# A fused retention, top-1 expert and top-2 attention kernel: the gathers behind the experts wait for tile halves, places are turned sooner, constants are multiplied in TensorE's waits

## The reference, cut to what matters

```python
# 1: retention, 8 heads of 64
for t in range(S):
    state = gamma * state + outer(k[:, :, t], v[:, :, t])
    y[:, :, t] = scale * q[:, :, t] @ state
# 2: one expert of 8 per token; a token keeps the expert of the one before it unless it is "fresh"
for b in range(B):
    for s in range(S):
        fresh_e = argmax(logits[b, s])
        e = fresh_e if s == 0 or local_gate[b, s] < 0.5 else prev_e
        prev_e = e
        out[b, s] = softmax(logits[b, s])[e] * (relu(x[b, s] @ w1[e]) @ w2[e])   # 512 -> 1024 -> 512
# 3: causal attention in each of 4 experts (head width 64), the best 2 of them mixed for each token
for e in range(4):
    a = softmax(causal(scale * (x @ wq[e]) @ (x @ wk[e]).T))
    out += weight_of_e_in_top2 * (a @ (x @ wv[e]) @ wo[e])
```

## Time and profile before

| | |
|---|---|
| median of 3 runs | 441.63 us (440.08 to 442.58) |
| the profiled execution | 441.96 us, of which the span of its instructions 440.4 us |
| PE busy | 400.6 us (91%), 3,224 matmul records |
| PEld | 357.2 us (81%) |
| DVE | 250.3 us (57%) |
| ACT | 230.3 us (52%) |
| POOL | 79.0 us (18%) |
| chain that ended last | PE 74%, issue 10%, DMA 7% |

### The profile page before, as it was taken

The page is one execution under the profiler, slowest core; times in us unless marked ns, Lnnn a source line. Parts: engine busy times, 40 slices in busy tenths (PEclk is TensorE's granted clock), DMA queues, the critical chain, the costliest instruction groups (busy, mean ns, idle before and its releaser), DMA issues.

```text
span 440.4 us, 9525 instructions
## 1 busy us (share of the span) xinstructions
PE 400.6 (91%) x3224; PEld 357.2 (81%) x3225; DVE 250.3 (57%) x483; ACT 230.3 (52%) x502; POOL 79.0 (18%) x100
## 2 busy tenths in 40 slices
PE   6999995397999999999999996599899899989987
PEld 5888783296999999999989895499787789978875
DVE  1576778775474746464646454335877441586740
ACT  4866665154464646464646462135666452466643
POOL 1011112011010101010000000730288300025330
PEclk9999998589999999999999999599999999999999
DMA  8958795777877776767767921542200030220003
GB/s 267 347 187 278 248 392 185 243 254 244 287 260 248 262 258 237 279 240 264 250 202 267 328 102 45 150 137 74 71 1 2 2 115 29 71 71 0 0 0 143
DMA packets 32354, 77.55 MB, mean 176 GB/s; under 512 B 3834, under 2 KB 4090, under 8 KB 32330
## 3 DMA queue, kind: packets, MB, share of 16 engines
q1 hardware_dynamic: 25642, 58.28, 39.2%
q0 software_dynamic: 4224, 14.68, 9.7%
q10 hardware_dynamic: 2464, 4.27, 2.7%
HBM read 56.18 MB, written 17.89 MB: 168 GB/s over the span
## 4 chain that ended last, share of the span: by engine, by line
PE 74%; issue 10%; DMA 7%; POOL 2%; DVE 2%; ACT 2%; SPq 1%; POOLq 1%; ACTq 0%; DVEq 0%
PE bank L1239 7%; PE bank L1240 7%; PE bank L1241 7%; PE bank L1226 6%; PE bank L1224 6%; PE bank L1225 6%; PE bank L1343 5%; PE bank L1328 5%; PE bank L1310 3%; PE bank L1314 3%; PE bank L1285 3%; PE bank L1284 3%; PE bank L1286 3%; POOL tokens_by_expert L448 2%; DMA tokens_by_expert<-zero 2%
## 5 line engine op out<-in xcount | busy, mean ns | idle before, releaser
L1224 PE MATMUL bank<-xh,w1h 128*128 128x240 f32 x256 | 71.1, 278 | 0.9 <-DVE xl L904 0.9
L1225 PE MATMUL bank<-xl,w1h 128*128 128x240 f32 x256 | 70.9, 277 | 0.0
L1226 PE MATMUL bank<-xh,w1l 128*128 128x240 f32 x256 | 70.8, 277 | 0.0
L898 DVE TENSOR_TENSOR w2l<-raw,w2h 128x1024 fp32r<-128x1024 f32 x32 | 37.2, 1221 | 42.7 <-ACT w2h L582 42.6
L582 ACT ACTIVATE w2h<-raw 128x1024 fp32r<-128x1024 f32 x32 | 31.7, 1051 | 47.8 <-PE bank L1241 45.7
L1239 PE MATMUL bank<-w2h,hh 128*128 128x512 f32 x128 | 50.6, 395 | 0.0
L1224 PEld LDWEIGHTS bank<-xh,w1h 128*128 128x128 f32 x256 | 49.4, 193 | 1.3 <-DVE xl L904 1.0
L499 POOL TENSOR_SCALAR att<-att,stat,mixw 128x128 f32<-128x128 f32 (+5 forms) x48 | 34.1, 719 | 88.9 <-DVE stat L1054 88.9
L1240 PE MATMUL bank<-w2l,hh 128*128 128x512 f32 x128 | 49.9, 390 | 0.0
L1241 PE MATMUL bank<-w2h,hl 128*128 128x512 f32 x128 | 49.8, 389 | 0.0
L1225 PEld LDWEIGHTS bank<-xl,w1h 128*128 128x128 f32 x256 | 49.4, 193 | 0.3
(11 more groups left out here) (161 smaller groups left out, 863.3 us busy)
## 6 DMA issues: line engine op xcount, KB each, us to landing
raw<-in_w SPq DMA_DIRECT2D x64, 512.0 KB, 6.2
tokens_by_expert<-zero POOLq DMA_DIRECT2D x8, 512.0 KB, 6.5
xr<-tokens_by_expert POOLq DMA_DIRECT2D x8, 512.0 KB, 4.2
kt_in<-in_kT SPq DMA_DIRECT2D x12, 256.0 KB, 4.9
q_in<-in_qT SPq DMA_DIRECT2D x12, 256.0 KB, 3.5
out<-osb SPq DMA_DIRECT2D x12, 256.0 KB, 2.0
outputs_by_expert<-zero SPq DMA_DIRECT2D x6, 480.0 KB
v_in<-in_vR SPq DMA_DIRECT2D x11, 256.0 KB, 4.2
```

What stands on the lines that cost most here:

```text
L898: dve.tensor_tensor(part(low), raw[:, q, :], part(high).bitcast(F32), ALU.subtract).then_inc(w_lo, 1)
L1224: pe.matmul(to, w1h[:, dc, at], xh[:, dc, 0:TILE], start=(dc == 0), stop=False)
L1225: pe.matmul(to, w1h[:, dc, at], xl[:, dc, 0:TILE], start=False, stop=False)
L1226: last = pe.matmul(to, w1l[:, dc, at], xh[:, dc, 0:TILE], start=False, stop=(dc == DC - 1))
```

## The change

- **Places.** Behind the last block TensorE multiplies the places of group 4 before the gates of block 11, and VectorE reads them before it counts group 5.
- **Constants.** TensorE multiplies constants (or weights that lie there) into PSUM bank 0, which nobody reads: two fp32 products of 256 columns behind the last gates, two behind the places of group 5, sixteen (`BUSY`) behind the counts, two (`BETWEEN`) behind the small product of the tile offsets; and ten and four fp32r products of 512 columns (`STILL`) ahead of the first and the second turning at the attention layer's entry.
- **Value products** follow the turning by one block, and not by two.
- **Padding.** GpSimd waits for SyncE's `first_padded` behind its own padding store, ahead of the tile load.
- **Stores.** Each half has its own semaphore `ey_stored[th]`. The zero stores (seven instead of six) have another, `ys_cleared`, for which ScalarE waits once, before the first expert. ScalarE no longer waits for all stores at the end: GpSimd does.
- **Gathers.** The last expert's count at the end of sequence 0 is kept (`seq_count`, `seq_row`), and VectorE works out for each half how many tiles have to be stored before sequence 0 can be gathered (`seq_i`). GpSimd reads these two numbers and waits for them; behind the six gathers it waits for all stores and raises `all_stored`, for which ScalarE and VectorE wait ahead of the attention's loop.

```diff
@@ -37,9 +37,12 @@
...
 WARM = 6
+BUSY = 16
+BETWEEN = 2
+STILL = (10, 4)
 GROUPS = ((0, 2), (2, 4), (4, 6), (6, 8), (8, 10), (10, 11), (11, 12))
 GMAX = 2
-CLEARED = MAX_TILES - E
+CLEARED = MAX_TILES - E + 1
@@ -54,7 +57,9 @@
...
 C_PADMIN = C_PICK + 1 + E
-C_N = C_PADMIN + E
+C_HALVES = C_PADMIN + E
+MAXH = -(-S // TILE)
+C_N = C_HALVES + TH * MAXH
@@ -96,6 +101,8 @@
...
     small[:, C_PADMIN] = TW
+    small[:, C_HALVES:C_HALVES + TH * MAXH] = (TILE * np.arange(MAXH)[None, :] + P * np.arange(TH)[:, None]).reshape(-1)
+    small[:, C_HALVES] = -1.0
     return decay.astype(np.float32), small.astype(np.float32)
@@ -139,6 +146,10 @@
...
         over = sb("over", [1, E * MAXT])
+        seq_count = sb("seq_count", [E, 1])
+        seq_row = sb("seq_row", [1, 1 + TH])
+        seq_over = sb("seq_over", [1, TH * MAXH])
+        seq_i = sb("seq_i", [1, TH], I32)
         ones = sb("ones", [E, GMAX * P])
@@ -241,7 +252,10 @@
...
         ey_done, ey_ready = sem("ey_done"), sem("ey_ready")
-        ey_stored, all_stored = sem("ey_stored"), sem("all_stored")
+        ys_cleared, all_stored = sem("ys_cleared"), sem("all_stored")
+        ey_stored = [sem(f"ey_stored{th}") for th in range(TH)]
+        seq_counted, seq_step, seq_ready, seq_stored = (
+            sem("seq_counted"), sem("seq_step"), sem("seq_ready"), sem("seq_stored"))
         delta_ready, pos2_step, pos2_ready = (
@@ -397,9 +411,9 @@
...
             sp.wait_ge(zeroed, 1)
-            for g in range(E, MAX_TILES):
-
-                sp.dma_start(rows(ys, g * TILE, TILE).rearrange("(p a) n -> p (a n)", p=TILE // 2), zero[0:TILE // 2, :]).then_inc(ey_stored, 16)
+            for g in range(MAX_TILES - CLEARED, MAX_TILES):
+
+                sp.dma_start(rows(ys, g * TILE, TILE).rearrange("(p a) n -> p (a n)", p=TILE // 2), zero[0:TILE // 2, :]).then_inc(ys_cleared, 16)
             for s in range(XRING):
@@ -457,7 +471,6 @@
...
             pool.wait_ge(first_tile_in, 16)
-            pool.wait_ge(first_padded, 16)
             pool.wait_ge(route_ready, 1)
@@ -471,16 +484,23 @@
...
                         pool.wait_ge(padded, 16 * e + 16)
+                        pool.wait_ge(first_padded, 16)
                     pool.wait_ge(tileT_done, 2 * g + 2)
                     load_tile(r)
+                return tb, nt
...
                 expert_loads(e, True)
-            expert_loads(E - 1, False)
+            tb, nt = expert_loads(E - 1, False)
             pool.wait_ge(pos2_ready, 1)
-            pool.wait_ge(all_stored, 1)
+            pool.wait_ge(seq_ready, 1)
+            tiles = [pool.value_load(seq_i[0:1, th:th + 1], min_val=E - th, max_val=MAX_TILES) for th in range(TH)]
+            for th in range(TH):
+                pool.wait_ge(ey_stored[th], 16 * tiles[th] + 16)
+            pool.sem_inc(seq_stored, 1)
+            pool.wait_ge(seq_stored, 1)
             def gather(b):
@@ -490,6 +510,10 @@
...
             gather(0)
+            for th in range(TH):
+                pool.wait_ge(ey_stored[th], 16 * (tb + nt) + 16)
+            pool.sem_inc(all_stored, 1)
+            pool.wait_ge(all_stored, 1)
             gather(1)
@@ -592,21 +616,24 @@
...
-                act.wait_ge(ey_stored, 16 * CLEARED + 16 * TH * (n - 1))
                 for th in range(TH):
                     live = min(P, TILE - th * P)
+                    act.wait_ge(ey_stored[th], 16 * n)
                     act.wait_ge(ey_done, TH * (n - 1) + th + 2)
...
                                              "there are at most MAX_TILES tiles, and n is at least one")
-                    act.dma_start(rows(ys, row, live), ysb[0:live, th, :]).then_inc(ey_stored, 16)
+                    act.dma_start(rows(ys, row, live), ysb[0:live, th, :]).then_inc(ey_stored[th], 16)
...
             act.activation(exps[:, :, :], exps[:, :, :], ACT.Exp).then_inc(exps_ready, 1)
+            act.wait_ge(ys_cleared, 16 * CLEARED)
+            for th in range(TH):
+                act.sem_inc(ey_stored[th], 16)
@@ -637,8 +664,6 @@
...
             tile_out(act.snap(tb + nt))
-            act.wait_ge(ey_stored, 16 * CLEARED + 16 * TH * (tb + nt))
-            act.sem_inc(all_stored, 1)
@@ -650,11 +675,12 @@
...
-            for t in range(C + 2):
+            for t in range(C + 1):
                 if t < C:
                     split_x2(0, t)
-                if t >= 2:
-                    values(0, t - 2)
+                if t >= 1:
+                    values(0, t - 1)
+            act.wait_ge(all_stored, 1)
             with act.Fori(0, B) as b:
@@ -818,6 +844,8 @@
...
                     dve.wait_ge(places_done, g - 1)
+                if g == closing[C - 1]:
+                    dve.tensor_copy(seq_count[:, :], cnt[:, s, w - 1:w]).then_inc(seq_counted, 1)
                 dve.scalar_tensor_tensor(post[:, s, 0:w], cnt[:, s, 0:w], cst[0:E, C_EBASE:C_EBASE + 1], sel[:, s, 0:w],
@@ -848,10 +876,10 @@
...
             last = len(GROUPS) - 1
+            read_places(last - 2)
             count_places(last - 1)
...
             fresh_choice(last)
-            read_places(last - 2)
             read_places(last - 1)
@@ -903,6 +931,7 @@
...
+            dve.tensor_copy(seq_row[:, 0:1], bank[0:1, 6, 2 * E - 1:2 * E]).then_inc(seq_step, 1)
             for q in range(4):
@@ -933,6 +962,15 @@
...
                                      ALU.add).then_inc(pos2_ready, 1)
+
+            dve.wait_ge(seq_step, 1)
+            dve.tensor_tensor(seq_over[:, :], seq_row[:, 0:1].to_broadcast([1, TH * MAXH]),
+                              cst[0:1, C_HALVES:C_HALVES + TH * MAXH], ALU.is_gt).then_inc(seq_step, 1)
+            dve.wait_ge(seq_step, 2)
+            dve.reduce_sum(seq_row[:, 1:1 + TH], seq_over[:, :].rearrange("o (h k) -> o h k", h=TH), AX.X).then_inc(seq_step, 1)
+            dve.wait_ge(seq_step, 3)
+            dve.tensor_tensor(seq_i[:, :], seq_row[:, 1:1 + TH],
+                              route_f[:, R_TB + E - 1:R_TB + E].to_broadcast([1, TH]), ALU.add).then_inc(seq_ready, 1)
@@ -974,6 +1012,7 @@
...
                 split_x2(0, t)
+            dve.wait_ge(all_stored, 1)
             with dve.Fori(0, B) as b:
@@ -1183,15 +1222,24 @@
...
                     block_kv(i)
+            def keep_clock(n):
+
+                for _ in range(n):
+                    pe.matmul(bank[:, 0, 0:2 * P], ident, cst[:, 0:2 * P], start=True, stop=True)
+
             last_g = len(GROUPS) - 1
             turn_fresh(last_g - 1)
+            turn_places(last_g - 2)
             rows_and_gates(NB - 1)
-            turn_places(last_g - 2)
+            keep_clock(2)
             turn_fresh(last_g)
             turn_places(last_g - 1)
+            keep_clock(2)
             turn_places(last_g)
             ends = (GROUPS[last_g][1] - GROUPS[last_g][0]) * P
+            pe.wait_ge(seq_counted, 1)
             pe.wait_ge(cnt_ready, last_g + 1)
+            pe.matmul(bank[0:1, 6, E:2 * E], seq_count[:, :], ident[0:E, 0:E], start=True, stop=True)
             pe.matmul(bank[0:1, 6, 0:E], cnt[:, last_g % 2, ends - 1:ends], ident[0:E, 0:E], start=True, stop=True).then_inc(counts_done, 1)
@@ -1204,11 +1252,13 @@
...
+            keep_clock(BUSY)
             pe.wait_ge(first_tile_in, 16)
...
             pe.matmul(bank[:, 7, 0:E], ones[0:1, 0:P], over[0:1, 0:E], start=True, stop=True).then_inc(ey_done, 1)
+            keep_clock(BETWEEN)
             pe.wait_ge(spare_set, 2)
@@ -1263,13 +1313,15 @@
...
-            for t in range(C + 2):
+            for t in range(C + 1):
+                for _ in range(STILL[t] if t < len(STILL) else 0):
+                    pe.matmul(bank[:, 0, :], hh[:, 0, 0:P], w2h[:, 0, :], start=True, stop=True)
                 if t < C:
                     turn_x2(0, t)
-                if t == 2:
+                if t == 1:
                     pe.wait_ge(m2_lo, 2)
-                if t >= 2:
-                    project_values(0, t - 2)
+                if t >= 1:
+                    project_values(0, t - 1)
             pe.wait_ge(masks_set, 2)
```

## The result

The changed kernel takes 435.23 us (median of 4 runs, 434.74 to 435.92), the kernel before 441.0 beside it (440.08 to 442.58); the ratio is 0.9867, 95% interval 0.9832 to 0.9901 (it is formed from runs beside each other, and need not be the quotient of the two medians). That is 5.8 us faster. The forecast was 429.0, a gain of 12 from there, and its range ended at 434: the direction was right, the size was not.

What follows compares the result with a forecast made beforehand. TensorE was taken as the bound nearly everywhere, with gains only where it waits or runs at half clock: routing to second expert tile (5.2 us) and experts' end (7.7). Together 12.9 off 441.96 gave 429.0 us, range 426.5 to 434.

Steps and rivals of the forecast that it cites:

- Part 1: End of routing: places turned sooner let the last scatter start earlier; 0.4 us taken, bounds 0 and 0.8.
- Part 2: Ahead of the first expert tile: fillers keep TensorE's clock up, so the first layer ends 3.1 us sooner.
- Rival (a): Fillers ahead of the first tile start at half clock and end late: 430.7 us, about 435.7 if slow throughout; chance 0.20.
- the sign of being wrong: Second expert tile waits for its load as long as before, or a new wait follows the gathers.
- Part 3: Second expert tile: GpSimd's earlier padding store lets its load go sooner, taking 5 us; its transposes come 5.2 us earlier.
- Rival (b): Second tile's load shares the DMA engines, takes its old 8.2 us, lands at 100.3: 432.1 us; chance 0.11.
- the first place: Stretch from routing to the second expert tile, where TensorE waits or runs at half clock; forecast gain 5.2 us.
- Part 4: End of experts: gathers wait only for halves holding sequence 0; first gather starts at 270.45 instead of 275.88, 5.4 us.
- The sign given: End of experts: first gather seen at about 265.3 in the changed profile, 270.45 less 5.2.
- Rival (c): End of experts: first gather still waits for the second half, so nothing gained there: 436.4 us; chance 0.03.
- Part 5: Attention layer's entry: fillers and shorter lag keep the clock; projections 7.7 us sooner, 5.4 from the gather, 2.3 the clock.

Runs made afterwards that it cites:

- e1: Changed kernel with GpSimd's wait for SyncE's first padding put back ahead of its own padding store; 438.85 us, ratio 0.9918.
- e3: Changed kernel with SyncE's w1 loads for expert 1 held until the second tile's rows have landed; 434.29 us, ratio 0.9824.
- e10: Changed kernel with the second padding store issued early by SyncE behind the first tile's load, GpSimd's later ones an expert further ahead; 427.66 us, ratio 0.9737.
- a_again: The changed kernel once more, nothing altered; 434.72 us, ratio 0.9898.
- e8: Changed kernel with old order of places, no fillers ahead of the first tile and the padding wait put back; gathers' changes stay; 433.39 us, ratio 0.9854.
- b_again: The kernel before once more, nothing altered, for a second profile; 444.2 us in one run.
- e4: Changed kernel without the constant products around the first tile (two, two, sixteen and two); 439.19 us, ratio 0.9874.
- e6: Changed kernel with the first gather waiting for all halves of all tiles, as in the kernel before; 444.88 us, ratio 1.0034.
- e9: Changed kernel with the value products again two blocks behind the turned blocks instead of one; 437.46 us, ratio 0.9943.
- e2: Changed kernel with each GpSimd padding store one expert further ahead, the first before its wait for the first tile; 433.62 us, ratio 0.9799.
- e7: Changed kernel with GpSimd's paddings one expert further ahead and no constant products around the first tile; 435.41 us, ratio 0.9794.

## Why the prediction was wrong, point by point

- **Part 1** (taken 0.4 us, 0 to 0.8): the step came, and then brought nothing. From xT to the last scatter it is 6.69 us (66.84 to 73.53), before 7.54 (69.38 to 76.92): 0.85, just over the upper bound. But the scatter then took 3.79 us and not 2.99, and the first tile was turned 14.3 us behind xT, as before. In e1 and e3 the scatter took 2.87 and 3.15, and the tile came at 13.5 and 13.6. Why it was slower in the changed profile, no run shows.
- **Part 2**, fillers: right in mechanism. The clock reads 1.00 through them, sixteen and their neighbours end at 80.3 and the tile comes 0.8 us behind; the first layer starts 2.72 us behind the first transposes (81.14 to 83.86; 2.62 forecast). Rival (a) didn't come. TensorE was ready for the second tile 28.0 us behind xT, before 30.4: 2.4 us of the 3.1 forecast (the rest is part 1's 0.4, and a first layer of 11.0 us instead of 10.8). They were won and then lost: TensorE was ready at 94.9 and waited 5.30, twice the 2.56 of before. The prediction had named just that as the sign of being wrong.
- **Part 3 is the step that failed**, in three terms. The padding store had bounds of 4.2 and 6.2 us and took 7.53: the forecast added two for "the weight loads in flight", and the store ran beside four w2 loads that had started only 4.0 us before it (80.09; 6.35 us before it in the old trace). The w1 loads were left at "about 93", their old place, though they follow the same first tile and moved with it, to 90.89. And so the tile load, issued at 92.45 within its bounds, didn't go ahead of them: 5 us taken, 7.68 measured, near the other end (8.2). It landed at 100.13, forecast 97.2. The end of the forecast's own bounds (93.3 + 8.2 = 101.5) held it; the choice within them, "because most of the weight loads start behind it", was wrong in its reason: two of the four were issued ahead of it. What ended the wait instead was that load beside its neighbours: e3 takes the neighbours away and it takes 4.15 us, with 1.78 of wait.
- **What the wait did to the clock** was in no term. A rest of 5.30 us before the second tile cost about 1 us in its transposes (1.97 against 1.10 in the earlier trace rows and 0.87 for the third) and slowed the products until about 104.7 (0.43 us from one to the next, then 0.23). From the second tile's transposes to the third's it is 24.8 us (100.18 to 124.95) where e10 takes 22.5 (94.74 to 117.26): 2.3 us, the last of the gain (1.4 in a_again's profile, 23.9 us). The kernel before isn't safe from it either: behind rests of 2.56 us in its first profile and 2.81 in e8 the second tile's transposes ran at the full clock (1.10 us), behind 2.51 in b_again and 2.91 in e4 at the half one (1.97), which is most of why the third tile of the kernel before stands at 55.5 in one profile and at 57.4 in the other. Rival (b) had the landing right (100.3) but not the store and not the clock: 2.1 us left for the first place, 432.1 in all; in truth nothing was left. The Trainium skill's rule that it drew on (Trainium Kernel Development and Optimization, Key Constraints: transfers from the three queues run on the same 16 DMA engines and interleave) fits what e3 shows here: 7.68 us beside the weight loads, 4.15 without.
- **Part 4**, the gathers: right. The first gather went at 270.31, forecast 270.45. (The sign given, 265.3, took the first place's 5.2 us off, which didn't come; the last expert tile was turned at 259.99 in both profiles.) e6 shows that it rests on the first half. Rival (c) didn't come.
- **Part 5**: mechanism right, size 1.2 us short (7.7 forecast, 6.5 measured). Its first transposes came at 274.25, forecast 274.5. The term that failed is the spacing of blocks, taken as 1.46 us from the old gathers, so that a step of TensorE, 1.88, was the bound: the third and fourth steps took 2.51 and 2.14, 0.9 of the 1.2. The third gather was issued at 272.90, 0.16 us behind the last half's store (272.74), and took 5.24 us against 3.48. In a_again, e8, e9 and e10, issued as close behind that store, it took 4.8 to 5.4. That the store is the reason isn't shown: other gathers are in flight beside it too, and no run takes the store away.
- **What the first place can give.** With the load out of the weights' way e10 has a span 5.7 us shorter than e8, which lacks the first place (431.9 and 426.2), and 5.7 by the medians; forecast 5.2. e10's ratio of 0.9737 is near the forecast's 0.9714 (429.0 of 441.63), but it is no merit of the forecast: the kernel that was forecast lacks the step that e10 adds.

## What to carry to other kernels

An edit that starts one transfer earlier moves everything that hangs on the same release: lay out anew who is in flight beside each transfer before its duration is carried over from the old trace. A transfer that the engine waits for should be issued ahead of those of the same size that nobody waits for yet; freeing its predecessor early helps only when both get out of their way. Two edits that each fill a wait of one place are worth only what the latest of its releasers allows, so ask for the place's other releaser first.

## What the runs showed of the hardware

The price of a transfer of 512 KB by its neighbours. The second tile's load took 4.15 us with no weight load beside it (e3). It took 5.2, 6.5 and 7.2 (e10, e2, e7) where it was issued ahead of the w1 loads and had the w2 loads and GpSimd's next padding store beside it. It took 6.71 to 9.05 in the ten profiles in which it starts 0.6 to 2.0 us behind the first w1 load (least in e1, most in e4). The padding store took 4.24 to 5.08 (before, b_again, e1) when it starts 6.3 to 6.5 us behind the first w2 load, 5.85 at 6.0 us (e8), and 6.88 to 7.67 at 4.0 to 4.3 us, in the seven others.

Some waits have no releaser in the kernel; the profile writes "remote". VectorE's in e2, of 2.4 and twice 1.5 us during the retention, and ScalarE's in the value products; then the same place in e4:

```profile
44.35 1.23 DVE L773 TENSOR_TENSOR probs<-bank,lead 128x1024 f32<-128x1024 f32 x1 [2.43 <-remote]
...
54.44 0.42 DVE L793 TENSOR_TENSOR state_sum<-bank,state 128x256 f32<-128x256 f32 x1 [1.57 <-remote]
...
276.69 0.39 ACT L678 ACTIVATE vg<-bank 128x260 f32<-128x260 f32 x1 [2.87 <-remote]
```

```profile
285.98 0.39 ACT L676 ACTIVATE vg<-bank 128x260 f32<-128x260 f32 x1 [2.98 <-PE bank L1313]
```

VectorE's three stand at the same places in before, b_again and e1 to e7, and in none of the other five profiles (changed, a_again, e8 to e10). The changed profile's head start at xT grows where they stand: its `xT` operation is 0.2 us ahead of before's ahead of the first wait (40.18 and 40.41), 1.1 behind it (45.62 and 46.68), 1.3 behind the second (56.01 and 57.31) and 2.5 behind the third. Since a_again shows none of them either, while e1 to e7, made from the same code there, do, they go with the group of runs (or its chip: the first two groups ran on one, the third on another) and not with the kernel. ScalarE's stands in e1, e2, e3 and e7. In e4 the profile names TensorE's last product of the block, but that had ended at 284.07, 1.9 us before: the same delay under another name. The tails of e1 to e4 are 1.8 to 2.0 us longer for it than the changed kernel's (e7's is 3.4 us longer). The kernel before shows none of it in b_again, nor e6, so the ratios of e1 to e4 and e7 may be some 0.4% too high; whether their other runs have it isn't known. What causes either wait isn't known; a reader should take such a wait off before comparing two profiles.
